# Attention and a gated MLP on one core: full-array matmuls on zero-padded heads, reciprocals in PSUM, and a new division of the small work

## What is computed

```python
k_sum = k.reshape(B, H, nb, 32, D).max(axis=3)
v_sum = v.reshape(B, H, nb, 32, D).mean(axis=3)
scores_l = where(abs(i - j) < 16, scale * q @ k.T, -1e9)
scores_s = scale * q @ k_sum.T + log(32)
a = softmax([scores_l, scores_s])
x = a @ [v, v_sum]                                # (2, 768, 512) over all heads
x = (sigmoid(causal_conv5(x)) * (x @ w_val)) @ w_out
h = relu(x @ w_in); u, v = h[..., :512], h[..., 512:]
v_s = w_spatial @ layernorm(v) + b_spatial
out = (u * v_s) @ w_out2
```

## Time and profile before

| | us |
|---|---|
| median of 3 timed runs | 350.4 |
| lowest and highest of them | 345.94, 353.49 |
| profiled execution, its own time | 343.46 |
| profiled execution, span from first to last instruction | 341.7 |
| TensorE busy | 321.6 (94%) |
| VectorE busy | 212.5 (62%) |
| ScalarE busy | 151.6 (44%) |
| GpSimd busy | 116.5 (34%) |

### The profile page before, as it was taken

One profiled execution on the slowest core, in us unless ns is written; L12 is line 12 of the kernel. 1 busy time (PEld: TensorE's weight loads), 2 busy tenths in 40 slices (PEclk: granted clock), 3 DMA queues, 4 the chain that ended last, 5 costly groups with the idle time before them and its releaser, 6 DMA issues.

```text
span 341.7 us, 5466 instructions
## 1 busy us (share of the span) xinstructions
PE 321.6 (94%) x1876; PEld 268.5 (79%) x1876; DVE 212.5 (62%) x628; ACT 151.6 (44%) x416; POOL 116.5 (34%) x121
## 2 busy tenths in 40 slices
PE   8599897888999999979999999999999999999997
PEld 8465564555666589867999999988889999998886
DVE  3688999999999999698793000078886433330000
ACT  2467795766888863632224222253332311112222
POOL 3006419447132024993038000034347733231000
PEclk9879999996999999998999999999999999999999
DMA  8896894577152122331000000022121000001222
GB/s 183 152 199 117 193 209 117 122 180 167 29 119 65 64 61 84 117 92 49 0 0 2 1 0 2 0 62 78 31 62 33 0 2 0 0 2 63 110 106 92
DMA packets 49465, 25.33 MB, mean 74 GB/s; under 512 B 43914, under 2 KB 44190, under 8 KB 49054
## 3 DMA queue, kind: packets, MB, share of 16 engines
q1 hardware_dynamic: 49438, 24.99, 29.6%
HBM read 21.24 MB, written 3.15 MB: 71 GB/s over the span
## 4 chain that ended last, share of the span: by engine, by line
PE 66%; DVE 14%; issue 7%; POOL 5%; DMA 3%; ACT 2%; SPq 1%; DVEq 0%; POOLq 0%
PE psum L577 54%; DVE neg_s L825 4%; PE psum L516 3%; POOL g_lo L445 3%; DVE probs L842 2%; DMA v_blk<-in_v_dram 2%; POOL win_v_lo L445 2%; PE psum L546 2%; PE psum L542 2%; PE psum L499 2%; DVE gate L885 2%; DVE sums_eps L831 1%; PE psum L660 1%; DVE k_max L856 1%; PE psum L524 1%
## 5 line engine op out<-in xcount | busy, mean ns | idle before, releaser
L445 POOL TENSOR_TENSOR g_lo<-work,g_hi 128x384 fp32r<-128x384 f32 x32 | 36.2, 1148 | 46.9 <-ACT g_hi L805 26.0
L704 ACT ACTIVATE probs<-neg_s,neg_max 128x184 f32<-128x184 f32 x96 | 42.1, 442 | 18.2 <-DVE neg_max L825 17.8
L842 DVE TENSOR_SCALAR probs<-probs,recip 128x184 f32<-128x184 f32 x96 | 45.7, 518 | 1.7
L516 PE MATMUL psum<-k_win,qT 64*128 64x184 f32 x192 | 30.0, 391 | 12.9 <-DVE neg_max L825 12.5
L885 DVE SCALAR_TENSOR_TENSOR gate<-xT,conv_c,gate 128x384 f32<-128x384 f32 (+8 forms) x44 | 40.7, 933 | 1.3
L445 POOL TENSOR_TENSOR vn_lo<-work,vn_hi 128x512 fp32r<-128x512 f32 x12 | 15.5, 1295 | 57.1 <-DVE vn_hi L1019 57.1
L516 PEld LDWEIGHTS psum<-k_win,qT 64*128 64x128 f32 x192 | 15.5, 197 | 20.8 <-DVE neg_max L825 16.1
L825 DVE CUSTOM_DVE_ANT_0 neg_s<-psum,mask 128x184 f32<-128x184 f32 x96 | 29.3, 341 | 2.2 <-PE psum L516 2.1
L718 ACT ACTIVATE probsT<-psum 128x384 f32<-128x384 f32 x48 | 23.4, 487 | 14.3 <-PE psum L526 14.2
L997 DVE TENSOR_TENSOR wsp_lo<-psum,wsp_hi 128x384 fp32r<-128x384 f32 x12 | 6.6, 548 | 33.6 <-ACT wsp_hi L786 33.6
L1029 DVE TENSOR_TENSOR work<-psum,b_row 128x384 f32<-128x384 f32 x16 | 8.9, 558 | 28.2 <-PE psum L577 26.6
(11 more groups left out here) (121 smaller groups left out, 756.9 us busy)
## 6 DMA issues: line engine op xcount, KB each, us to landing
k_nat<-in_k_dram SPq DMA_DIRECT2D x16, 192.0 KB, 3.2
q_nat<-in_q_dram SPq DMA_DIRECT2D x16, 192.0 KB, 3.8
v_blk<-in_v_dram SPq DMA_DIRECT2D x4, 768.0 KB, 8.2
v_nat<-in_v_dram SPq DMA_DIRECT2D x16, 192.0 KB
out_dram<-work SPq DMA_DIRECT2D x11, 256.0 KB, 2.0
raw<-in_moe_w_spatial_dram SPq DMA_DIRECT2D x6, 384.0 KB, 3.0
raw<-in_moe_w_out_dram SPq DMA_DIRECT2D x8, 256.0 KB, 2.8
raw<-in_moe_w_in_dram SPq DMA_DIRECT2D x8, 256.0 KB, 2.7
```

What stands on the lines that cost most here:

```text
L445: nc.gpsimd.tensor_tensor(dst_lo, src, dst_hi.bitcast(F32), ALU.subtract).then_inc(lo_sem, 1)
L516: ins = nc.tensor.matmul(bank_s(i, h), qT[d, s, t * P:(t + 1) * P], k_win[d, s, t, KEYS[h]], start=True, stop=True)
L704: ins = nc.scalar.activation(probs[:, i % 4, w], neg_s[:, i % 3, w], ACT.Exp, bias=neg_max[:, i % 4, h:h + 1], scale=-1.0, accum_out=sums[ ...
L842: ins = nc.vector.tensor_scalar(a, a, recip[:, i % 4, h:h + 1], None, ALU.mult)
```

## The change

- Queries go into `qT` of both heads, with zeros in the other head's 64 rows; values into `v_main` with 64 zero columns between the heads. All score and value matmuls then use the full array of 128 rows and 128 columns, and the value matmuls of both heads accumulate into the same output. The transposes of probabilities are full too.
- A step's scores of both heads go into one PSUM bank, two banks in turn; the wait moves from one step behind to two. `turn_probs` comes 5 steps behind and `values` 6 (before 3 and 4), with six `probs` buffers.
- Sums and reciprocals are made once for two steps; 1e-9 lies in a column of `sums`, the reciprocals are written to PSUM, and `normalise` is one multiplication of both heads by a broadcast of them.
- `k` and `q` are turned in three pieces of 256 columns, one a step, through two banks. VectorE copies `k` and the second head's `q`, ScalarE the first head's.
- GpSimd's queue has a new order, by pair: `mean_v`, convolution taps of gates 0 and 1, `k_tails`, then both parts of x and of a `w_val` piece. VectorE keeps the convolution of gate 2, at the end of attention.
- Four `val` products lie in the last steps instead of two; the banks are numbered anew.

In the excerpt, "..." marks lines left out. Of the main loops, `add_eps`, `invert_sums` and `normalise` only the new lines stand here; their old ones are those of the kernel above.

```diff
-            return psum[:, (2 * i + h) % 3, 0:HEAD]
-        bank_t = psum[:, 3, 0:3 * P]
-        bank_qk = psum[:, 4:6, :].rearrange("p a n -> p (a n)")
+            return psum[:, i % 2, h * HEAD:(h + 1) * HEAD]
+        bank_t = psum[:, 2, 0:3 * P]
+        def recip(i):
+            return psum[:, 3, i % 4 * 2:i % 4 * 2 + 2]
+        def bank_qk(n):
+            return psum[:, 4 + n % 2, 0:PIECE]
...
-                    sp.wait_ge(used, p - n + 1)
+                    sp.wait_ge(used, PIECES * (p - n + 1))
...
-                    sp.dma_start(v_nat[:, s, :, d], x).then_inc(done, 16)
+                    sp.dma_start(v_main[:, s, :, 2 * h * D:(2 * h + 1) * D], x).then_inc(done, 16)
...
+                pool.wait_ge(xT_ready, T // 2 * (p + 1))
+                nc.gpsimd.tensor_copy(x_hi[:, p, :], xT[:, p, :]).then_inc(x_hi_ready, 1)
                 split(x_hi[:, p, :], x_lo[:, p, :], xT[:, p, :], x_hi_ready, p + 1, x_split)
+            def split_wval(n):
+                wait_piece(pool, n)
+                nc.gpsimd.tensor_copy(wval_hi[:, n, :], raw[:, n % 3, 0:DM]).then_inc(wval_hi_ready, 1)
+                split(wval_hi[:, n, :], wval_lo[:, n, :], raw[:, n % 3, 0:DM], wval_hi_ready, n + 1, w_split)
...
+            def conv_tap(n):
...
+                term, acc = gate[:, C - 1, m:S], gate[:, p, m:S]
+                nc.gpsimd.tensor_scalar(term, xT[:, p, 0:S - m], w, None, ALU.mult).then_inc(early_conv, 1)
+                pool.wait_ge(early_conv, before + 1)
+                nc.gpsimd.tensor_tensor(acc, acc, term, ALU.add).then_inc(early_conv, 1)
...
+            nc.gpsimd.memset(qT[:, 0, :, :], 0.0).then_inc(q_zeros, 1)
             make_mask()
+            nc.gpsimd.memset(qT[:, 1, :, :], 0.0).then_inc(q_zeros, 1)
             k_tails(0)
-            for i in range(STEPS):
-                p, t = divmod(i, T)
-                if t == 2 and p + 1 < PAIRS:
+            for p in range(PAIRS):
+                if p % 2 == 0 and p // 2 + 1 < PAIRS // 2:
+                    mean_v(p // 2 + 1)
+                for n in CONV_OF[p]:
+                    conv_tap(n)
+                if p + 1 < PAIRS:
                     k_tails(p + 1)
-                if t == 3 and p % 2 == 0 and p // 2 + 1 < PAIRS // 2:
-                    mean_v(p // 2 + 1)
-                if t == 4 and 1 <= p <= W_OUT:
-                    split_w(p - 1, wval_hi[:, p - 1, :], wval_lo[:, p - 1, :])
-                if t == 5 and 1 <= p:
+                if p >= 1:
                     split_x(p - 1)
+                if 1 <= p <= W_OUT:
+                    split_wval(p - 1)
...
+            def turn_k(p, piece):
+                if piece < 2 and p >= 1:
+                    pe.wait_ge(qA_ready, PIECES * (p - 1) + 2 + piece)
+                    pe.wait_ge(qB_ready, PIECES * (p - 1) + 2 + piece)
+                elif piece == 2:
+                    pe.wait_ge(kT_ready, PIECES * p + 1)
+                turn(k_nat, p, piece, k_loaded, k_turned)
+            def turn_q(p, piece):
+                if piece < 2:
+                    pe.wait_ge(kT_ready, PIECES * p + 2 + piece)
+                else:
+                    pe.wait_ge(qA_ready, PIECES * p + 1)
+                    pe.wait_ge(qB_ready, PIECES * p + 1)
+                turn(q_nat, p, piece, q_loaded, q_turned)
...
-                if i >= 1:
-                    pe.wait_ge(masked, 2 * i - 1)
+                if t % 2 == 0:
+                    pe.wait_ge(qA_ready, PIECES * p + t // 2 + 1)
+                    pe.wait_ge(qB_ready, PIECES * p + t // 2 + 1)
+                if i >= 2:
+                    pe.wait_ge(masked, 2 * (i - 1))
                 for h in range(2):
-                    d = slice(h * D, (h + 1) * D)
-                    ins = nc.tensor.matmul(bank_s(i, h), qT[d, s, t * P:(t + 1) * P], k_win[d, s, t, KEYS[h]],
+                    ins = nc.tensor.matmul(bank_s(i, h), qT[:, s, h, t * P:(t + 1) * P], k_win[:, s, t, KEYS[h]],
...
-                nc.tensor.matmul(o[0:D], v_nat[:, s, t, 0:D], pT[:, 0:P], start=True, stop=False,
-                                 skip_group_check=True)
-                nc.tensor.matmul(o[D:P], v_nat[:, s, t, D:P], pT[:, P:2 * P], start=True, stop=False,
-                                 skip_group_check=True)
-                nc.tensor.matmul(o, v_rest[0:2 * SIDE, s, t, :], pT[0:2 * SIDE, 2 * P:3 * P], start=False, stop=True,
-                                 skip_group_check=True).then_inc(x_summed, 1)
+                nc.tensor.matmul(o, v_main[:, s, t, 0:P], pT[:, 0:P], start=True, stop=False)
+                nc.tensor.matmul(o, v_main[:, s, t, D:D + P], pT[:, P:2 * P], start=False, stop=False)
+                nc.tensor.matmul(o, v_rest[:, s, t, :], pT[:, 2 * P:3 * P], start=False,
+                                 stop=True).then_inc(x_summed, 1)
...
+                if p + 1 < PAIRS:
+                    if t < PIECES:
+                        turn_k(p + 1, t)
+                    else:
+                        turn_q(p + 1, t - PIECES)
+                if p == PAIRS - 1 and 1 <= t <= C:
+                    turn_wout(t - 1)
+                if STEPS + 1 <= i < STEPS + 1 + VALS_IN:
                     val(i - STEPS - 1)
+                if 5 <= i < STEPS + 5:
+                    turn_probs(i - 5)
+                if 6 <= i:
+                    values(i - 6)
...
+                nc.scalar.activation(qT[0:D, p % 2, 0, piece * PIECE:(piece + 1) * PIECE],
+                                     bank_qk(PIECES + piece)[0:D], ACT.Copy).then_inc(qA_ready, 1)
...
+            for i in range(STEPS + 7):
                 p, t = divmod(i, T)
+                if 5 <= i < STEPS + 5:
+                    take_probsT(i - 5)
+                if p + 1 < PAIRS and t >= PIECES:
+                    turned_q(p + 1, t - PIECES)
                 if i < STEPS:
                     exponentials(i)
+                if i >= 8 and i % 2 == 0:
+                    take_x((i - 8) // 2)
+                if 1 <= i - (PAIRS - 1) * T <= C:
+                    turned_wout(i - (PAIRS - 1) * T - 1)
+                if (p, t) == (6, 1):
+                    make_gate(0)
...
+            def add_eps(j):
+                dve.wait_ge(exp_done, 2 * j + 2)
+                i = 2 * j % RING
+                nc.vector.tensor_reduce(sums_eps[:, j % 2, :, :], sums[:, i:i + 2, :, :], AX.X, ALU.add).then_inc(
                     eps_added, 1)
+            def invert_sums(j):
+                dve.wait_ge(eps_added, j + 1)
+                nc.vector.reciprocal(psum[:, 3, j % 2 * 4:j % 2 * 4 + 4],
+                                     sums_eps[:, j % 2, :, :].rearrange("p a h -> p (a h)")).then_inc(recip_ready, 1)
             def normalise(i):
+                dve.wait_ge(recip_ready, i // 2 + 1)
+                a = probs[:, i % RING, :].rearrange("p (h n) -> p h n", h=2)
+                r = recip(i).rearrange("p (h n) -> p h n", n=1).broadcast_to((P, 2, HEAD))
+                nc.vector.tensor_tensor(a, a, r, ALU.mult).then_inc(probs_ready, 1)
...
+                dve.wait_ge(k_turned, PIECES * p + piece + 1)
+                nc.vector.tensor_copy(k_win[:, p % 2, 2 * piece:2 * piece + 2, MAIN:MAIN + P],
+                                      bank_qk(piece).rearrange("p (t k) -> p t k", k=P)).then_inc(kT_ready, 1)
...
+                nc.vector.tensor_copy(qT[D:P, p % 2, 1, piece * PIECE:(piece + 1) * PIECE],
+                                      bank_qk(PIECES + piece)[D:P]).then_inc(qB_ready, 1)
...
+            for i in range(STEPS + 4):
                 p, t = divmod(i, T)
+                if i >= 4:
+                    normalise(i - 4)
                 if i == 0:
                     add_blocks(0)
                 if i == 1:
...
                                             ALU.mult).then_inc(v_mean_ready, 1)
                 if i < STEPS:
                     mask_scores(i, 0)
+                if i % 2 == 1 and 3 <= i < STEPS + 3:
+                    add_eps((i - 3) // 2)
+                if i < STEPS:
                     mask_scores(i, 1)
+                if p + 1 < PAIRS:
+                    if t < PIECES:
+                        turned_k(p + 1, t)
+                    else:
+                        turned_q(p + 1, t - PIECES)
+                    if 1 <= t <= PIECES:
+                        max_k(p + 1, t - 1)
+                    if t == PIECES + 1:
+                        sum_k(p + 1)
+                if i % 2 == 1 and 3 <= i < STEPS + 3:
+                    invert_sums((i - 3) // 2)
+                if 1 <= i - (PAIRS - 1) * T <= C:
+                    split_wout(i - (PAIRS - 1) * T - 1)
+                if STEPS - 1 <= i < STEPS - 1 + TAPS:
+                    conv(ATT_GATES, i - (STEPS - 1))
...
+RING = 6
+VALS_IN = 4
+CONV_OF = ((), (), (), range(0, 3), (), range(3, 5), range(5, 8), range(8, 10))
```

More of the change, by code:

```diff
@@ L137, in attention_gated_mlp @@
         v_zeros = sem("v_zeros")
+        q_zeros = sem("q_zeros")
+        eps_set = sem("eps_set")
```

(53 more changed lines are left out.)

228 lines of the change are left out of this document (86 added, 142 removed).

## The result

The changed kernel takes 386.9 us (median of 4 runs, 385.1 to 388.9) against 348.2 (4 runs, 343.0 to 353.5) for the kernel before on the same chip: a ratio of 1.123, 95% interval 1.110 to 1.137. The profiled execution took 385.05 us, its span 383.3, its mean granted clock 0.938 (0.975 before). Each group of experiments was measured beside the kernel before on one chip, where that kernel's medians were 342 to 345 us; so the ratio is what compares, and differences in us between kernels of different groups are good to some 3 us.

The account below looks back on a forecast made before the run. VectorE was taken to bound attention, TensorE right behind; with three waits for key tails, steps of 1.95 us and a 14.1 us tail, attention ends at 158.9 instead of 130.8, so runs take 378 us, range 361 to 392.

Parts of the forecast that it names:

- three idle stretches of 9 to 12 us: TensorE idle ahead of the first scores of pairs 1, 3 and 5, released by GpSimd's second copy into `k_win`.
- The order: GpSimd's queue: `mean_v` ahead of `k_tails` makes the next pair's tails hang on a 768 KB load, three times.
- step 6: First scores of pair 1: load landed at 28.4, tree and mean 6.2, tails 0.75, start at 35.4 us (34.5 to 37).
- step 18: First scores of pair 3: 23.5 us after the turn in step 11 (21.3 to 25), at 71.6 us.
- The step: One attention step: TensorE 1.84 us, VectorE 1.82, taken as 1.95 (1.84 to 2.3) against 2.39 before.
- Lost packing: Rival on TensorE: full-array matmuls stay 0.42 apart, 2.97 us a step, 407 us in all; chance 0.04.
- The multiplication: VectorE's `normalise`, one multiplication over 368 elements with a PSUM operand: 0.50 us (0.45 to 0.56), whatever GpSimd does.
- For a copy or product by a scalar of 768 [...] I take 1.0.: GpSimd's added operations of 768 elements: 1.0 us each, ends 0.7 and 1.81.
- the block of pair 3: GpSimd's splits, weights, taps and tails behind step 18: 12.4 us against 11.7 for six steps; fits or costs 1.
- the deeper lag: `turn_probs(i-5)` and `values(i-6)`: only lets VectorE run late and lengthens the tail of attention.
- In later pairs it fits: GpSimd's added work in the pairs after pair 3 fits into the time of the steps.
- Nothing comes back: Stage behind attention is GpSimd's, 23.6 us; four `val` products in the tail only make TensorE wait longer there.

Follow-up runs that it names:

- the half-width experiment: Kernel with taps on VectorE, later `w_out` splits and two `val` products, its first two value matmuls made 64 wide and packed again: 339.1 us, ratio 0.991.
- The exchange of the tile: Reciprocals in an SBUF tile instead of PSUM, against the kernel with taps on VectorE and later `w_out` splits: 353.1 us, ratio 1.027.
- the circle through `woutT_hi`: Mask, exponentials, `woutT_hi`, VectorE's split; opened by splitting `w_out` one step later, against the kernel with taps on VectorE: 342.0 us, ratio 0.994.
- the first expectation: For the changed kernel with `k_tails` first in GpSimd's loop, then mean_v, splits, taps last: expected 335 to 340 us, measured 362.6, ratio 1.050.
- the fastest version: Changed kernel with tails first, taps on VectorE, `w_out` splits one step later and two `val` products in the tail: 337.8 us, ratio 0.984.

## Why the prediction came out as it did

The direction, the range and the main mechanism held: a tree that hangs on a load stands ahead of the tails, and TensorE waits. But of the three idle stretches of 9 to 12 us that were named, two came (11.8 and 10.1 us, ahead of pairs 1 and 3); the one ahead of pair 5 was 2.6, and three came that were not named (7.4, 5.3 and 4.3, ahead of pairs 4, 6 and 7). Attention ended 12.2 us later than forecast (171.1, where the last value matmul ends, against 158.9): up to step 30 the sum was 5.6 us too large, from there on 17.8 too small. That the median came within 9 us of 378 has a share of luck. The profiled execution was forecast at 371.5 and took 385.05, 13.5 more; the 7 us that were added because the median before lay above its profiled execution were 1.9 in the changed kernel, and this hid 5 us of the error.

- *The order.* "Tree, then tails", with TensorE waiting at step 6 and step 18: shown by the timelines and by both kernels that move only the tree. Step 6 started at 32.1 (forecast 35.4), since the load had landed at 25.6 and not at 28.4. The turn in step 11 was done at 44.0 (forecast 48.0) and step 18 started at 66.15 (forecast 71.6); between them lie the issues (8.5 us, 8.4 taken), the landing (7.0, 8.2 taken) and tree and tails (6.5, 6.95 taken). These terms were 5.4 us too large in all. The lower clock cost 1.7 to 1.9 us in the first step behind each wait of 5 us and more, against 2 taken.
- *The step.* 1.84 at 2.4 GHz as worked out from "without changes of shape"; the 1.95 taken in the sum was too careful. Lost packing, the rival of 407 us, fell: scores start 0.16 apart, and the half-width experiment shows the sign for the values.
- *The multiplication.* 0.53 against 0.50 taken, inside its ends, and independent of GpSimd. The exchange of the tile shows that PSUM does this, for 11 us. (The average of 0.95 us a step for the old pair of multiplications is the group's busy 45.7 us over 48 steps; 96 x 518 ns, which the prediction names for it, would be 1.04, since the two of a pair overlap.)
- *"For a copy or product by a scalar of 768 [...] I take 1.0."* This term failed. The copies take 0.82 to 0.88, but the product by a scalar takes 2.2 (75.17 in the timeline above), above even the upper end of 1.81. And the block of pair 3 was forecast at 12.4 us, "fits or costs 1". It had two gaps of the same size: the five operations of 1.8 to 2.4 take 10.7 where 6.7 was taken, and the splits could not start at once behind the tails but waited 4.4 for ScalarE's `xT`. For that wait the prediction had no term: "the deeper lag [...] only lets VectorE run late and lengthens the tail", while in fact `take_x`, which now copies outputs seven and eight steps behind, came to stand behind the step that the tails release. The block took 20.1, and a wait of 7.4 came ahead of pair 4. "In later pairs it fits" failed the same way: pairs 6 and 7 waited, and the 12 steps from step 30 to step 42 took 34.9 us (102.1 to 137.0) instead of 25.4: +9.5. No run separates the two gaps.
- *Where one wait shortened another.* The wait ahead of pair 4 cost nothing by step 30. The turn in step 23 was done at 78.1 (forecast 84.2), and from there to step 30 it took 24.0 us, as forecast (23.5): issues, landing, tree and tails. While TensorE stood still for the tails of pair 4, SyncE went through the transfers of the next pair (78.13 to 86.66) up to the load of the next tree (issued at 86.66 in its timeline), so TensorE's wait ahead of pair 5 was 2.6 us and not 10.8. The first of these two waits took the place of most of the second.
- *The last pair.* From step 42 to the end of attention 34.1 us against 25.8: +8.3. The prediction did not look for the circle through `woutT_hi`, 7 us when it was opened. The four `val` products in the tail it did count, and rightly as not coming back; two fewer gave 4.2.
- *Behind attention.* "Nothing comes back": 24.7 us from attention's end to the end of `win_v_lo` (195.8), 23.6 before; +41.6 in span for +40.3 in attention.

What fell besides was a thought of the first expectation rather than of the sum: that with the order mended the change would end 2 to 4% below the kernel before. For 1.6% it needed the taps off GpSimd (13.6 us), the circle opened (7.0) and two products moved back (4.2) as well. Left open: how the fastest version divides its remaining time; between 24 and 110 us VectorE is busy 81.3 us and TensorE 79.8 of 86, so both are near their end.

## What to carry to other kernels

In an in-order queue, ask of each block which engine stands still until the queue is past it, and put that engine's few short operations ahead of everything that hangs on a load or takes long; then sum the queue's work between two such operations and compare it with the bound engine's pace, because work beyond that has to go to another stretch or another engine. Look too for what the queue itself waits for: here GpSimd's block began with data that another queue held behind the very step which the block before had to release. A faster bound engine should make every such deadline earlier: the same misplaced tree cost 3.6% at steps of 2.39 us, and 19 us (some 5%) at steps of 1.84 with the taps beside it; no run separates the pace from the taps. Price an operation by a row of the same kind: a product by a per-partition scalar was costed from a copy, and 36.7 us of taps stood where some 25 were taken.

## What the runs showed of the hardware

- On GpSimd a TENSOR_SCALAR over 128x768 float32 with a per-partition scalar took 2.21 us, more than a TENSOR_TENSOR of the same size (1.80) and 2.7 times a CAST to the matmul format (0.82). On VectorE the corresponding groups have means of 0.83 for the first tap and 1.35 for those with an addition in the same instruction.
- VectorE's TENSOR_TENSOR over 368 elements takes 0.53 us with its second operand in PSUM or in SBUF, but only with both in SBUF is it held up by GpSimd: up to 2.27 us (beside the tree of adds), where its longest with one in PSUM is 0.54.
- After waits of 5.3 to 11.8 us TensorE resumed at 1.2 GHz (granted clock 0.50 to 0.54 in the first step). After one of 4.3 us ahead of pair 7 it resumed at the upper level, as its scores of 0.89 us show, and then fell: 0.50 from 138.3 to 141.0. After one of 2.6 us ahead of pair 5 the granted clock stayed at 1.00.
